# Diagonal term of a linear attention: from TensorE transposes and sums to token-layout products on GpSimd and VectorE

## The reference, cut to what matters

```python
batch, n_heads, seq, head_dim = (4, 8, 768, 48)
for t in range(S):
    kt, vt, rt = (k[:, :, t], v[:, :, t], r[:, :, t])
    cur = np.einsum('bhd,bhe->bhde', u[None] * kt, vt)
    y[:, :, t] = np.einsum('bhd,bhde->bhe', rt, state + cur)
    state = w[None, :, :, None] * state + np.einsum('bhd,bhe->bhde', kt, vt)
x = y in token rows, 3072 x 384
logits = x @ w_gate                # 8 experts, 384 tokens each, chosen in the order of the logits
out[mask] = relu(x[mask] @ w1[e]) @ w2[e]
return (a * b) @ w_out             # a = out @ w_a, b = out @ w_b
```

## Time and profile before

| | |
|---|---|
| Median of 3 runs | 857.12 us (857.03 to 857.69) |
| The profiled execution | 858.88 us |
| Its span | 856.6 us, granted clock 0.984 in the mean |
| PE busy | 834.4 us (97%), 7144 instructions |
| PEld busy | 797.6 us (93%) |
| DVE busy | 480.3 us (56%), 1297 instructions |
| ACT busy | 232.8 us (27%), 500 instructions |
| POOL busy | 306.9 us (36%), 320 instructions |
| DMA | 61.71 MB |

### The profile page before, as it was taken

How to read it: one execution, slowest core, us unless ns; L and a number is a source line. 1 busy time by engine, 2 the same in 40 slices (tenths; PEclk the granted TensorE clock), 3 DMA queues, 4 the chain that set the end, 5 groups by cost and what they waited for, 6 DMA issues and landing times.

```text
span 856.6 us, 17839 instructions
## 1 busy us (share of the span) xinstructions
PE 834.4 (97%) x7144; PEld 797.6 (93%) x7144; DVE 480.3 (56%) x1297; ACT 232.8 (27%) x500; POOL 306.9 (36%) x320
## 2 busy tenths in 40 slices
PE   8999996699999999999999999999999999999997
PEld 6999995599999999999999999999999999999997
DVE  7676668666655565556655665566556422641321
ACT  2333330232321232223222232223222322322222
POOL 5588872120381038102810282027202820381001
PEclk9999997599999999999999999999999999999999
DMA  9999950400230023002300240014001400230000
GB/s 170 225 220 234 219 135 31 156 20 1 75 102 28 1 74 104 28 1 67 110 29 1 63 114 29 1 53 124 29 1 50 127 28 1 72 105 28 1 1 28
DMA packets 102209, 61.71 MB, mean 72 GB/s; under 512 B 79344, under 2 KB 92144, under 8 KB 102128
## 3 DMA queue, kind: packets, MB, share of 16 engines
q1 hardware_dynamic: 94976, 46.43, 21.6%
q0 software_dynamic: 3072, 9.44, 3.5%
q10 hardware_dynamic: 4080, 4.72, 1.6%
HBM read 51.13 MB, written 9.44 MB: 71 GB/s over the span
## 4 chain that ended last, share of the span: by engine, by line
PE 95%; DVE 2%; DMA 1%; issue 1%; POOL 1%; ACT 0%; POOLq 0%; DVEq 0%; ACTq 0%
PE bank L1722 43%; PE bank L1813 17%; PE bank L1780 12%; PE bank L1493 3%; PE bank L1515 3%; PE bank L1793 2%; PE bank L1504 2%; PE bank L1471 2%; PE bank L1758 1%; PE bank L1481 1%; PE bank L1542 1%; PE bank L1527 1%; PE bank L1711 1%; PE bank L1797 1%; PE bank L1553 1%; PE bank L1567 1%
## 5 line engine op out<-in xcount | busy, mean ns | idle before, releaser
L1722 PE MATMUL bank<-act,w_all 128*128 128x384 f32 x1584 | 294.4, 337 | 0.0
L1722 PEld LDWEIGHTS bank<-act,w_all 128*128 128x128 f32 x1584 | 274.5, 188 | 0.0
L631 POOL TENSOR_TENSOR w<-wst,w 128x384 fp32r<-128x384 f32 (+1 forms) x100 | 134.4, 1349 | 362.8 <-ACT w L1410 356.5
L1813 PE MATMUL bank<-w_all,gs 128*128 128x384 f32 x855 | 167.3, 339 | 0.0
L1813 PEld LDWEIGHTS bank<-w_all,gs 128*128 128x128 f32 x855 | 148.3, 188 | 0.2 <-DVE gs L1263 0.2
L1254 DVE TENSOR_TENSOR bank<-ga,bank 128x384 f32<-128x384 f32 x95 | 54.8, 577 | 107.3 <-PE bank L1722 93.2
L1780 PE MATMUL bank<-hs,w 128*128 128x384 f32 x576 | 112.0, 339 | 0.0
L1780 PEld LDWEIGHTS bank<-hs,w 128*128 128x128 f32 x576 | 99.4, 189 | 0.0
L1722 PE MATMUL bank<-act,w 128*128 128x384 f32 x504 | 98.9, 339 | 0.0
L1440 ACT ACTIVATE gs<-bank 128x384 fp32r<-128x384 f32 x95 | 46.8, 492 | 171.5 <-DVE bank L1254 161.0
L1431 ACT ACTIVATE ga<-bank 128x384 f32<-128x384 f32 x96 | 47.2, 492 | 154.1 <-PE bank L1722 132.9
(11 more groups left out here) (250 smaller groups left out, 973.2 us busy)
## 6 DMA issues: line engine op xcount, KB each, us to landing
wst<-in_moe_w SPq DMA_DIRECT2D x48, 256.0 KB, 3.4
wst<-in_moe_w SPq DMA_DIRECT2D x58, 192.0 KB, 2.4
kt<-in_k SPq DMA_DIRECT2D x24, 192.0 KB, 4.3
rt<-in_r SPq DMA_DIRECT2D x24, 192.0 KB, 4.6
vt<-in_v SPq DMA_DIRECT2D x24, 192.0 KB, 4.9
x_rows<-xs ACTq DMA_DIRECT2D x24, 192.0 KB, 3.5
raw<-in_moe_w_a SPq DMA_DIRECT2D x6, 384.0 KB, 6.5
raw<-in_moe_w_b SPq DMA_DIRECT2D x6, 384.0 KB, 5.1
```

Source lines behind the costliest of these rows:

```text
L631: pool.tensor_tensor(lo, src, hi.bitcast(F32), ALU.subtract).then_inc(w_split, 1)
L1722: last = pe.matmul(dst, wt(a), mv(b), start=(n == 0 and (a, b) == (0, 0)), stop=(n == len(pairs) - 1 and (a, b) == (1, 0)))
L1813: last = pe.matmul(acc[t][:, 0:D], gs[:, a, t * P:t * P + P], wo2[:, b, c, :], start=(c == 0 and (a, b) == (0, 0)), stop=(c == FFC - 1 and ...
```

## The change

- The diagonal's sums are made in token layout: POOL multiplies r by u (`weigh_r`, into the new `ru`), DVE multiplies that in place by the keys (`weigh_k`) and sums each head's 48 products (`sum_heads`). `products`, `diagonals`, `copy_sums`, the table `uw` and PE's waits for them go. u is loaded by one DMA to all 128 partitions.
- The update's matmuls use 48 columns of `ktok`, not 64; rows 48 to 63 and 112 to 127 of its PSUM bank are set to zero once.
- Only the 12 raw pieces of w_a and w_b are split inside the attention (one in most tiles from 3 to 21); the 6 of w_out are split by ACT and POOL behind their last tile.

```diff
-            rk = at("rk", [P, 2, PAIRS, P])
+            ru_mem = at("ru_mem", [P, 2, PAIRS, P])
+            ru = [ru_mem[:, q, 0:DC, :].rearrange("p c t -> p (c t)").rearrange("p (h d) -> p h d", d=DH)
+                  for q in range(2)]
...
+        RAW_EARLY = 2 * DC * FF // PIECE
         def raw_step(p):
-            return 3 + p * (NT - 6) // (RAW_PIECES - 1)
+            return 3 + p * (NT - 6) // (RAW_EARLY - 1)
...
@@ sync
-                for p in range(RAWS, RAW_PIECES):
+                for p in range(RAWS, RAW_EARLY + RAWS):
                     if raw_step(p - RAWS) + 1 == n:
                         load_raw(p)
+            for p in range(RAW_EARLY + RAWS, RAW_PIECES):
+                load_raw(p)
...
@@ gpsimd
             pool.wait_ge(table_ready, 1)
-            pool.wait_ge(s_cdve, CD_ALL)
...
+            def weigh_r(n):
+                pool.wait_ge(in_landed[n % SLOTS], 48 * (n // SLOTS + 1))
+                if n >= 2:
+                    pool.wait_ge(dsum_ready, n - 1)
+                pool.tensor_tensor(ru[n % 2], rt[:, n % SLOTS, :, 0:DH], u_tok[:, :, :], ALU.mult
+                                   ).then_inc(ru_ready, 1)
...
-            for n in range(3):
-                scale_keys(n)
+            scale_keys(0)
+            scale_keys(1)
+            pool.wait_ge(u_landed, 16)
+            weigh_r(0)
+            scale_keys(2)
+            weigh_r(1)
+            pool.wait_ge(s_cdve, CD_ALL)
             for n in range(NT):
                 late_constants(n)
                 diagonal(n)
                 if (n + 1) % TPB:
                     fade(n + 1)
                 if n + 3 < NT:
                     scale_keys(n + 3)
-                lower_raw(n - 1)
+                if n + 2 < NT:
+                    weigh_r(n + 2)
+                lower_raw(raw_pieces(n - 1))
+            for p in range(RAW_EARLY, RAW_PIECES):
+                lower_raw([raw_part(p)])
...
@@ vector
-            def products(n):
-                dve.wait_ge(rs_ready, n + 1)
-                dve.wait_ge(ks_ready, n + 1)
+            def weigh_k(n):
+                dve.wait_ge(ru_ready, n + 1)
+                dve.tensor_tensor(ru[n % 2], ru[n % 2], kt[:, n % SLOTS, :, :], ALU.mult).then_inc(ruk_ready, 1)
+            def sum_heads(n):
+                dve.wait_ge(ruk_ready, n + 1)
                 if n >= 2:
-                    dve.wait_ge(diag_done, n - 1)
-                dve.tensor_tensor(rk[:, n % 2, :, :], rs[:, n % 3, :, :], pK, ALU.mult
-                                  ).then_inc(rk_ready, 1)
+                    dve.wait_ge(dv_ready, n - 1)
+                dve.tensor_reduce(dsum[:, n % 2, :], ru[n % 2], AX, ALU.add).then_inc(dsum_ready, 1)
...
                 scale_r(n + 2)
-                products(n + 2)
+                weigh_k(n + 2)
                 if n:
                     cut_scores(n + 1)
+                sum_heads(n + 2)
                 outputs(n)
...
@@ scalar
+            act.dma_start(u_tok[:, :, :].rearrange("p h d -> p (h d)"),
+                          u.rearrange("(o h) d -> o (h d)", o=1).to_broadcast([P, H * DH])).then_inc(u_landed, 16)
...
             store(NT - 1)
+            for p in range(RAW_EARLY, RAW_PIECES):
+                upper_raw([raw_part(p)])
...
@@ tensor
-                        last = pe.matmul(pU[HALVES[h2], a, :], ktok[:, n % 3, 2 * a + h2, :],
+                        last = pe.matmul(pU[h2 * HALF:h2 * HALF + DH, a, :], ktok[:, n % 3, 2 * a + h2, 0:DH],
                                          vt[:, n % SLOTS, 2 * a + h2, :], start=True, stop=True)
-            def diagonals(n):
...
             def x_turn(n):
                 pe.wait_ge(x_ready, n + 1)
-                if n < NT - 3:
-                    pe.wait_ge(dsum_ready, n + 2)
-                    if n >= 1:
-                        pe.wait_ge(lg_ready, n)
+                if 1 <= n < NT - 3:
+                    pe.wait_ge(lg_ready, n)
```

More of the change, by code:

```diff
@@ L385, in attention_moe_bilinear, with raw_part @@
         assert RAW_PIECES * PIECE == (B - 1) * SPAN
+        RAW_EARLY = 2 * DC * FF // PIECE
         def raw_step(p):
-            return 3 + p * (NT - 6) // (RAW_PIECES - 1)
+            return 3 + p * (NT - 6) // (RAW_EARLY - 1)
+        def raw_part(p):
+            return (p, raw[:, p % RAWS, :],
+                    w_all[:, p * PIECE // SPAN, :, p * PIECE % SPAN:p * PIECE % SPAN + PIECE])
         def raw_pieces(n):
-            return [(p, raw[:, p % RAWS, :],
-                     w_all[:, p * PIECE // SPAN, :, p * PIECE % SPAN:p * PIECE % SPAN + PIECE])
-                    for p in range(RAW_PIECES) if raw_step(p) == n]
+            return [raw_part(p) for p in range(RAW_EARLY) if raw_step(p) == n]
         HALVES = [slice(0, HALF), slice(HALF, P)]
@@ L570, in fade, with lower_raw @@
                                    ALU.mult).then_inc(state_ready, 1)
-            def lower_raw(n):
-                for p, piece, cols in raw_pieces(n):
+            def lower_raw(pieces):
+                for p, piece, cols in pieces:
                     pool.wait_ge(raw_hi, p + 1)
@@ L719, in _ @@
             step(last)
[L720 to L725, removed]
+            step(dve.memset(pU, 0.0))
             assert made[0] == CD_ALL
@@ L778, in _ @@
             scale_r(0)
-            products(0)
             scale_r(1)
@@ L782, in _ @@
             cut_scores(0)
-            products(1)
+            weigh_k(0)
             add_update(0)
+            sum_heads(0)
             hole_made = [0]
@@ L849, in _ @@
                     cut_scores(1)
-                products(n + 2)
+                    weigh_k(1)
+                    sum_heads(1)
+                weigh_k(n + 2)
                 if n:
                     cut_scores(n + 1)
+                sum_heads(n + 2)
                 outputs(n)
@@ L858, in _ @@
             scale_r(NT - 1)
-            products(NT - 1)
+            weigh_k(NT - 1)
             cut_scores(NT - 2)
+            sum_heads(NT - 1)
             outputs(NT - 3)
@@ L1323, in _ @@
             load_decay(act, 0)
-            act.wait_ge(s_fill, 2)
-            for h2 in range(2):
-                rows = slice(h2 * HALF, h2 * HALF + DH)
-                act.dma_start(u_col[rows, :, :], u[h2:H:2, :].rearrange("a (d o) -> d a o", o=1),
-                             allow_slow_non_contiguous=True).then_inc(s_u, 16)
+            act.dma_start(u_tok[:, :, :].rearrange("p h d -> p (h d)"),
+                          u.rearrange("(o h) d -> o (h d)", o=1).to_broadcast([P, H * DH])).then_inc(u_landed, 16)
             def copy_keys(n):
@@ L1360, in copy_logits, with upper_raw @@
                 act.activation(logit[:, n, :], pL, ACT.Copy).then_inc(lg_ready, 1)
-            def upper_raw(n):
-                for p, piece, cols in raw_pieces(n):
+            def upper_raw(pieces):
+                for p, piece, cols in pieces:
                     act.wait_ge(raw_landed[p % RAWS], 16 * (p // RAWS + 1))
@@ L1596, in _ @@
             update(0)
-            diagonals(0)
             for n in range(NT - 2):
@@ L1610, in _ @@
                     update(n + 1)
-                diagonals(n + 1)
                 if 1 <= n < NT - 3:
@@ L1614, in _ @@
             scores(NT - 1)
-            diagonals(NT - 1)
             from_state(NT - 2)
```

48 lines of the change are left out of this document (11 added, 37 removed).

## The result

| | before | after |
|---|---|---|
| Median | 857.08 us, 4 runs (856.12 to 857.69) | 906.26 us, 4 runs (903.98 to 907.65) |
| Ratio to before | | 1.0565, 95% interval 1.0541 to 1.0588 |
| The profiled execution | 858.88 us | 905.74 us |
| Its span, granted clock | 856.6 us, 0.984 | 904.0 us, 0.958 |

The change makes the kernel 49.2 us slower by the medians, 5.65% by the ratio. The forecast was 39 slower, 896 us with a range of 866 to 911.

The account below looks back on a forecast made before the run. PE bounds the kernel before up to about 137 us, then a DVE-POOL loop sets the attention's turns. Attention +29.7, start +2.6, end -1.1, routing stage +8 make +39.2 on 858.9: 898.1, predicted median 896 us, range 866 to 911.

Parts of the forecast that it names:

- the loop: Attention: fade waits for DVE's add_update, weigh_r stands behind fade and keys, DVE waits for weigh_r; 6.11 us a turn unblocked.
- the block and its overlap: Attention: weigh_k, with two SBUF inputs, waits for POOL's running instruction, begins 0.14 us before its end, finishes 0.41 behind.
- the end: Behind add_update(22): the last output and first digit masks come 1.1 us earlier (0 to -2).
- the routing stage: Behind the attention: six w_out pieces on POOL hold up DVE's small steps, +8 us (0 to 11.1).
- the attention: From add_update(1) to add_update(22): 140.4 us against 110.7 before, +29.7.
- The 14 single turns: Between add_update(1) and add_update(21): 7 with a raw piece, 6 without, one with a constant, 99.9 us together.
- The pairs at the batches' ends: Attention: three pairs of turns where a batch ends without update or fade, 12.5, 11.6 and 10.7, together 34.8 us.
- the last turn: Attention: the turn to add_update(22), which has no keys, takes 5.7 us.
- Rival 2: Attention: PE's clock falls in its idle stretches, on a quarter of 24 tiles, 15 us more: 911 us; chance 0.16.
- the start: Up to add_update(1): weigh_k of tiles 0, 1 and 2 delays it, +2.6 us (1.4 if nothing blocks).
- the step from the profiled execution to the median: Whole kernel: the profiled execution lies 1.8 us above the median, so 898.1 became 896 us.
- The terms for the gain: PE in the attention: diagonal matmuls gone, 10.8 us, and 48-column updates, 2.2; together 13.0 if PE stays the bound.

Follow-up runs that it names:

- without the block: The changed kernel with weigh_k's second input for 20 of 24 tiles taken from an idle PSUM bank, not SBUF, output wrong: 881.14 us, ratio 1.0272.
- PE kept busy: The changed kernel with 8 unneeded matmuls of 112 columns on PE ahead of each x_turn up to tile 20: 899.13 us, ratio 1.0489.
- the best version: The changed kernel with weigh_r ahead of the fade, 17 of 18 raw pieces, all inside the attention, on DVE, ACT's logit copy ahead of its store: 850.33 us.

## Why the prediction was right, and where its sum was short

**Right: the loop.** Turns without a raw piece take 6.62 us (the prediction had 6.67), with one 7.60 to 7.63 (7.69), without the block 6.00 (6.11). DVE and POOL wait for each other. Without the block the loop still sets a turn of 6.00; with `weigh_r` moved out of it the 14 turns take 5.05 us in the mean, block and all, and 44.4 us come back. The two runs together show it.

**Right: the block and its overlap.** `weigh_k` ended 0.42 us behind the raw piece, as computed from the one row of the routing stage. The rule of the Trainium skill, "SBUF — State Buffer" (who interferes with whom), names the right cause (two SBUF inputs against GpSimd's reads; the run with a PSUM input agrees), but its full block would have made it 0.55.

**Right: the end and the routing stage.** -1.0 for -1.1, and +8.9 for +8. The kernel before with the w_out pieces alone moved late is 9.2 slower.

**Short: the attention, +33.9 for +29.7.** The 14 single turns take 100.9 us for 99.9, with two that stand out: 7.07 for 6.67, where two of DVE's constants stand ahead of the update, and 7.43 for 6.11, the one shown above. The pairs at the batches' ends take 37.5 for 34.8 (12.4 for 12.5, 13.7 for 11.6, 11.3 for 10.7), the last turn 6.2 for 5.7. The step that failed is that PE's lower clock was put beside the sum as a rival, all or nothing. It comes behind some of the gaps, for part of a tile: 0.50 directly behind the one of 2.58 us above, while behind a gap of 2.20 us before 61.73 `x_turn` and the scores still ran at full clock (0.52 and 1.16 us) and only the groups from 63.27 on at half (the values took 1.89). The length of the gap alone does not tell: behind 1.58 us before 42.69 `x_turn` took 0.84, behind 1.57 before 36.07 it took 0.52. Where DVE is late anyway a low clock costs nothing, where PE's values are needed it cost 1.3. With PE kept busy the stretch takes 141.0, the prediction's own 140.4 and 0.6. That closeness is luck in part: the seven turns with a raw piece are 0.6 us shorter in sum than predicted, and the pairs 1.2 longer (36.0 for 34.8) at full clock too, which no run explains. Rival 2 had the right rows and four times the price: 15 us, where filling the gaps gave back 3.5 in the attention.

**Short: the start, +3.4 for +2.6.** Moving `weigh_r` takes 1.5 us of it back, the filled gaps 0.2; the rest no experiment separates.

**Left out: behind the gather, +2.2.** The prediction had nothing here. Between the first gather and the end the twelve other changed kernels have 696.5 to 699.3 us and before 698.8; after's 701.0, in one profile, is the longest. In the ten us from 213 on its clock is 0.64, where before has 0.85 at the same distance from its gather. The kernel with the pieces put back, whose attention has the same loop and gaps like after's, has 0.85 too, and 699.0. So the attention's gaps alone don't explain it; what does stays open.

**Left out: the step from the profiled execution to the median.** The prediction took 1.8 us off, since before's profiled execution lay that much above its median. After's (905.74) lies 0.5 below its own. Of the 10 us between 896 and 906.3, 8.2 are terms of the span and nearly all the rest is this step. The 1.8 was the scatter of one execution.

**The terms for the gain** were there: PE's diagonal and the 48 columns take 9.7 us off PE in the best version. In the change they bought nothing, since PE was no longer the bound.

## What to carry to other kernels

When work goes from the bound engine to two idle ones, draw the loop between them through each engine's order, not through the data: here the product needed nothing of the fade, and stood behind it all the same; two lines moved were worth 44 of 49 us. Give DVE at most one SBUF input where POOL always has something running, or put the longer of two such instructions on the faster engine. And a stage in which POOL is idle is no free place for its work if DVE's small steps are the path there.

## What the runs showed of the hardware that I had not expected

- Beside POOL's raw pieces DVE steps on 4 to 24 int32 numbers with one SBUF input (a scalar operation, a cast) took 1.3 to 1.8 us, where they take 0.17. In the prediction I had made two inputs the condition, though the copy of three columns has one. The Trainium skill, "SBUF — State Buffer" (who interferes with whom), counts copies, casts and scalar operations among those that can contend; the rows agree.
- The block works both ways: beside DVE's two-input instructions POOL's `dv` took up to 1.18 us for 0.83 in after, the keys 1.33 to 1.72 for 1.00 (the runs with `weigh_r` moved, the longest with 17 pieces on DVE), the fade 1.48 for 0.83 there.
- DVE's 128x768 difference takes 0.95 us and POOL's 1.83.
- PE's records with 48 weight columns follow each other in 22.5 ns, those with 64 in 29.
- Behind a gap of 2.58 us in a tile of 7.6 PE's clock stood at 0.50, though PE had been busy, at 1.00, up to the gap. It fell behind gaps of 1.58 us too (before 42.69), and not behind others of that length.
